# A linear-attention and two-MLP kernel: the first four jobs' odd key pairs turned by GpSimd, and their order on each engine changed

## The reference

```python
def _attn_ref(q, k, v, f_logit):            # (4, 8, 768, 48) each
    f = 1.0 / (1.0 + np.exp(-f_logit))
    for t in range(S):
        state = f[:, :, t, :, None] * state + np.einsum('bhd,bhe->bhde', k[:, :, t], v[:, :, t])
        y[:, :, t] = np.einsum('bhd,bhde->bhe', q[:, :, t], state)

def _moe_ref(x, w_in, w_out):               # (3072, 384) @ (384, 2048), and back
    r = np.maximum(x @ w_in, 0.0)
    return (r * r) @ w_out

def _moe2_ref(x, w_in, w_out):
    h = x @ w_in
    return (h * np.tanh(log1p(exp(h)))) @ w_out
```

## Time and profile before

| | |
|---|---|
| median of 3 runs | 886.29 us (885.81 to 890.02) |
| the profiled execution | 886.69 us, of which 885.0 us are the span from first to last instruction |
| PE busy | 874.3 us (99%) |
| DVE, ACT, POOL busy | 597.2, 594.8, 62.0 us |
| the chain that ended last | PE 98% |
| first instruction of `up1(0)` | 28.62 us from the span's start |
| granted TensorE clock | 1.000 |

### The profile page before, as it was taken

The page is one execution under the profiler, slowest core; times in us unless marked ns, Lnnn a source line. Parts: engine busy times, 40 slices in busy tenths (PEclk is TensorE's granted clock), DMA queues, the critical chain, the costliest instruction groups (busy, mean ns, idle before and its releaser), DMA issues.

```text
span 885.0 us, 16260 instructions
## 1 busy us (share of the span) xinstructions
PE 874.3 (99%) x6282; PEld 725.3 (82%) x6282; DVE 597.2 (67%) x1054; ACT 594.8 (67%) x1026; POOL 62.0 (7%) x71
## 2 busy tenths in 40 slices
PE   8899999999999999999999999999999999999998
PEld 7788888888888888888788888888888888888886
DVE  6879545445544444342244799999898898898886
ACT  6776655564546555544566787888887887877874
POOL 0222111111111111110000000000000000000000
PEclk9999999999999999999999999999999999999999
DMA  9644221122212111100233201001001001000100
GB/s 255 203 148 128 76 81 44 44 81 65 66 45 80 44 44 57 46 13 1 92 96 100 90 19 37 37 0 37 37 1 37 36 1 37 36 0 1 36 1 36
DMA packets 25090, 50.64 MB, mean 57 GB/s; under 512 B 2674, under 2 KB 3442, under 8 KB 25010
## 3 DMA queue, kind: packets, MB, share of 16 engines
q1 hardware_dynamic: 25010, 49.56, 18.0%
HBM read 40.11 MB, written 9.44 MB: 56 GB/s over the span
## 4 chain that ended last, share of the span: by engine, by line
PE 98%; DMA 1%; issue 0%; SPq 0%; ACT 0%; DVE 0%; ACTq 0%
PE ps L1069 45%; PE ps L1086 44%; PE ps L1043 2%; PE ps L1013 2%; PE ps L1039 2%; PE ps L991 1%; PE ps L1059 1%; DMA work<-fkq 1%; SPq L284 0%; PE ps L988 0%; PE ps L997 0%; SPq L297 0%; ACT work L497 0%; ACT work L538 0%; SPq L306 0%
## 5 line engine op out<-in xcount | busy, mean ns | idle before, releaser
L1069 PE MATMUL ps<-xs,w_hi 128*128 128x512 f32 x1152 | 359.3, 393 | 1.0 <-issue 1.0
L1069 PEld LDWEIGHTS ps<-xs,w_hi 128*128 128x128 f32 x1152 | 213.0, 188 | 45.0 <-issue 1.6
L1086 PE MATMUL ps<-g_hi,w_lo 128*128 128x512 f32 x576 | 224.1, 389 | 0.0
L1069 PE MATMUL ps<-xs,w_lo 128*128 128x512 f32 x576 | 224.1, 389 | 0.0
L1086 PE MATMUL ps<-g_hi,w_hi 128*128 128x512 f32 x576 | 224.1, 389 | 0.0
L1086 PE MATMUL ps<-g_lo,w_hi 128*128 128x512 f32 x576 | 224.1, 389 | 0.0
L829 DVE TENSOR_TENSOR g_lo<-gb,g_hi 128x512 fp32r<-128x512 f32 x96 | 68.1, 709 | 215.6 <-ACT gb L564 215.6
L559 ACT ACTIVATE rb<-ps 128x512 f32<-128x512 f32 x96 | 57.3, 597 | 161.0 <-PE ps L1069 161.0
L1069 PEld LDWEIGHTS ps<-xs,w_lo 128*128 128x128 f32 x576 | 108.1, 188 | 22.6
L1086 PEld LDWEIGHTS ps<-g_hi,w_hi 128*128 128x128 f32 x576 | 108.1, 188 | 22.5
L1086 PEld LDWEIGHTS ps<-g_hi,w_lo 128*128 128x128 f32 x576 | 108.1, 188 | 22.4
(11 more groups left out here) (82 smaller groups left out, 750.6 us busy)
## 6 DMA issues: line engine op xcount, KB each, us to landing
work<-fkq SPq DMA_DIRECT2D x68, 224.0 KB, 3.7
stage<-w SPq DMA_DIRECT2D x24, 384.0 KB, 3.1
work<-v_tok SPq DMA_DIRECT2D x22, 256.0 KB, 3.9
x_scratch<-yo SPq DMA_DIRECT2D x6, 768.0 KB, 3.8
xs<-x_scratch SPq DMA_DIRECT2D x6, 768.0 KB, 4.4
out<-work SPq DMA_DIRECT2D x17, 256.0 KB, 2.1
yo<-w SPq DMA_DIRECT2D x8, 384.0 KB, 4.6
work<-f_tok SPq DMA_DIRECT2D x4, 224.0 KB, 3.5
```

What stands on the lines that cost most here:

```text
L1069: ins = nc.tensor.matmul(bank, w[:, f, k * P:(k + 1) * P], xs[:, half, part, k, :], start=k == 0 and i == 0, stop=k == KT - 1 and i == 2)
L1086: ins = nc.tensor.matmul(ps[:, 5 + d, :], w[:, f, cols], g[:, slot, :], start=f == 0 and i == 0, stop=f == NF - 1 and i == 2)
```

## The change

What it does, by engine:

- PE: `keys(j)` of the first four jobs is four whole transposes; those of pairs 1 and 3 read `turned`, a copy of the pair with its halves swapped, and wait for `kt_turned`. `increments(j)` has two matmuls for each pair, of 64 and 48 columns, where it had four of 32 and 16 (for all 20 jobs that have increments). `idle_products` makes 2 and 1 matmuls of 384 moving columns, where it made 6 and 3 of 128. `scores(0)` goes ahead of `sums(2)`, `scores(1)` ahead of `sums(3)`, `scores(2)` ahead of `keys(2)` and `values(1)`, `increments(1)` ahead of `values(2)`.
- POOL: `turn(j)`, two copies of 112x2x64 elements for each of the four jobs, in `rb`. The second job's and later ones wait for `kT_done` of the job before, since `turned` is one buffer.
- ACT: `first_logarithm(2)` goes behind `first_decay(1)`; `keys_out(2)` and `keys_out(3)` go ahead of `weights_hi(0)` and `ends_out(2)`, and write in `eb`, so that they no longer wait for `kv_done`; `inverse_decay(4)` and `(5)`, which write over `eb`, wait for it instead.
- DVE: `first_cap(2)` goes behind `first_queries(0)`.

```diff
--- before.py
+++ after.py
@@ -34,7 +34,7 @@
     WF = 2 * DM
     NT = NF * NCH
     AHEAD = 4
-    IDLE = [6, 3]
+    IDLE = [(3, 3), (3,)]
     LIMIT = 8.0e16
     BOUND = 1.0e18
     CAP = 1.0e17
@@ -188,7 +188,7 @@
         names = """set_up zeroed st_zeroed const_ready causal_ready
             ft_exped ft_capped ft_logged sums_done m_ready
-            exped inv_f scanned logged p_ready ends_kept kt_ready gp_ready qp_ready qt_ready pc_ready
+            exped inv_f scanned logged p_ready ends_kept kt_ready kt_turned gp_ready qp_ready qt_ready pc_ready
             kT_done kT_out a_done a_out y_done kv_done s_added s_ready
             mx_kept mx_out mx_in mx_reduced flag_ready
             fsel_zeroed f_set_up f_loaded f_ready fv_loaded fkv_ready fst_ready fw_ready fy_done fy_out
@@ -239,11 +239,17 @@
         tri = rb[:, 0:C]
+        turned = rb[:, C:C + 2 * C].rearrange("p (n h t) -> p n h t", n=2, h=2)
         def f_rows(j):
             return (fb if j < 2 else eb)[:, j % 2, :, :].rearrange("p n t -> p (n t)")[:, 0:NP * R]
         def key_rows(j):
+            if j in (2, 3):
+                return eb[:, j % 2, :, :].rearrange("p n t -> p (n t)")[:, 0:NP * R].rearrange("p (n r) -> p n r", r=R)
             return ktT[:, j % 2, :, :]
         def v_rows(j):
@@ -480,6 +486,16 @@
                 nc.gpsimd.tensor_tensor(eb[0:R, j % 2, :, :], mb[0:R, j % 2, :, :], pb[0:R, j % 2, :, :],
                                         ALU.mult).then_inc(s_["gp_ready"], 1)
+            def turn(j):
+                pool.wait_ge(s_["kt_ready"], j + 1)
+                wait(pool, s_["kT_done"], j)
+                k = kt[0:R, j % 2, 1::2, :].rearrange("p n (h t) -> p n h t", h=2)
+                for h in range(2):
+                    nc.gpsimd.tensor_copy(turned[0:R, :, h, :], k[:, :, 1 - h, :]).then_inc(s_["kt_turned"], 1)
+            for j in range(B):
+                turn(j)
             for j in range(B, NJ):
                 decayed_keys(j)
                 residual(j)
@@ -514,6 +530,8 @@
                 act.wait_ge(s_["pc_ready"], j - 1)
                 act.wait_ge(s_["sums_done"], B)
                 act.wait_ge(f_in[j % 2], 16 * (j // 2 - 1))
+                if j < B + 2:
+                    act.wait_ge(s_["kv_done"], j - 1)
                 e = eb[0:R, j % 2, :, :]
                 nc.scalar.activation(e, fb[0:R, j % 2, :, :], ACT.Exp, scale=-1.0).then_inc(s_["exped"], 1)
                 act.wait_ge(s_["exped"], j - B + 1)
@@ -533,8 +551,6 @@
                 act.wait_ge(s_["kT_done"], j + 1)
                 if j >= B:
                     act.wait_ge(s_["kv_done"], min(j - 1, NJ - B))
-                elif j >= 2:
-                    act.wait_ge(s_["kv_done"], j - 1)
                 nc.scalar.activation(key_rows(j), ps_k(j), ACT.Copy).then_inc(s_["kT_out"], 1)
             def x1_hi(j):
@@ -650,9 +666,9 @@
             first_exponential(2)
             first_growth(0)
             first_decay(0)
-            first_logarithm(2)
             first_growth(1)
             first_decay(1)
+            first_logarithm(2)
             ends_out(0)
             first_exponential(3)
             first_growth(2)
@@ -664,15 +680,15 @@
             first_decay(3)
             keys_out(1)
             x1_hi(0)
+            keys_out(2)
             weights_hi(0)
             x1_hi(1)
+            keys_out(3)
             ends_out(2)
             ends_out(3)
             x1_hi(2)
             x1_hi(3)
             weights_hi(1)
-            keys_out(2)
-            keys_out(3)
             weights_hi(2)
             inverse_decay(4)
             for k in range(SPLIT):
@@ -901,9 +917,9 @@
             first_cap(0)
             first_cap(1)
-            first_cap(2)
             first_keys(0)
             first_queries(0)
+            first_cap(2)
             first_keys(1)
             first_queries(1)
             first_cap(3)
@@ -981,14 +997,13 @@
                     pe.wait_ge(s_["r1_ready"], 2)
                 if j == B + 1:
                     pe.wait_ge(s_["kT_out"], B + 1)
                 for n in (0, 2, 1, 3):
+                    k = kt[0:R, j % 2, n, :]
                     if j < B and n % 2 == 1:
-                        for at in (0, HC):
-                            ins = nc.tensor.matmul(ps_k(j)[at:at + HC, n, :], kt[0:R, j % 2, n, HC - at:C - at], ident[0:R, 0:R],
-                                                   start=True, stop=True, skip_group_check=True, tile_position=(0, at))
-                    else:
-                        ins = nc.tensor.transpose(ps_k(j)[:, n, :], kt[0:R, j % 2, n, :], ident[0:R, 0:R])
+                        if n == 1:
+                            pe.wait_ge(s_["kt_turned"], 2 * j + 2)
+                        k = turned[0:R, n // 2, :, :].rearrange("p h t -> p (h t)")
+                    ins = nc.tensor.transpose(ps_k(j)[:, n, :], k, ident[0:R, 0:R])
                 ins.then_inc(s_["kT_done"], 1)
             def sums(j):
@@ -1053,10 +1068,9 @@
                 else:
                     pe.wait_ge(s_["r1_ready"], begin[j + 1] + 1)
                 for n in range(NP):
-                    for i in range(4):
-                        lo, hi = Q * i, min(Q * i + Q, R)
-                        v0, v1 = VALUES[i // 2]
-                        ins = nc.tensor.matmul(ps_kv(j)[lo:hi, n, :], key_rows(j)[:, n, lo:hi], v_rows(j)[:, 2 * n + i // 2, v0:v1],
+                    for par, (lo, hi) in enumerate(ROWS):
+                        v0, v1 = VALUES[par]
+                        ins = nc.tensor.matmul(ps_kv(j)[lo:hi, n, :], key_rows(j)[:, n, lo:hi], v_rows(j)[:, 2 * n + par, v0:v1],
                                                start=True, stop=True, skip_group_check=True, tile_position=(0, lo))
                 ins.then_inc(s_["kv_done"], 1)
@@ -1144,31 +1158,32 @@
-            def idle_products(count, bank):
-                for i in range(count):
-                    nc.tensor.matmul(ps[:, bank, 0:P], ident[:, :], ident[:, :], start=True, stop=True, skip_group_check=True)
+            def idle_products(widths, bank):
+                for n in widths:
+                    nc.tensor.matmul(ps[:, bank, 0:n * P].rearrange("p (n t) -> p n t", t=P), ident[:, :],
+                                     ident[:, :].unsqueeze(1).to_broadcast([P, n, P]), start=True, stop=True, skip_group_check=True)
             pe.wait_ge(s_["const_ready"], 4)
             idle_products(IDLE[0], 6)
             sums(0)
             sums(1)
             idle_products(IDLE[1], 6)
+            scores(0)
             sums(2)
-            scores(0)
             keys(0)
+            scores(1)
             sums(3)
-            scores(1)
             keys(1)
             values(0)
+            scores(2)
             keys(2)
-            scores(2)
             values(1)
+            scores(3)
             keys(3)
-            scores(3)
             increments(0)
+            increments(1)
             values(2)
             values(3)
-            increments(1)
             increments(2)
             increments(3)
             for k in range(SPLIT):
```

## The result

The changed kernel is slower: 892.49 us median of 6 runs (891.16 to 893.47), beside 886.66 us of the kernel before (6 runs) on the same chip; ratio 1.0058 [1.0040, 1.0075]. The profiled execution took 892.25 us, of them 890.5 us of span. The forecast was 882.0, with 881.0 to 886.0. In all six runs the mean granted clock is 0.996 to 0.998.

What follows compares the result with a forecast made beforehand. TensorE's chain was taken as the bound, held ahead of `up1(0)` by instruction fetches and VectorE. `up1(0)` from 28.62 to 24.2 gives 4.4 us, so 881.9; with 0.1 for VectorE's slack 882.0, range 881.0 to 886.0.

Steps and rivals of the forecast that it cites:

- increments 64 to 32 by four: Instruction count ahead of `up1(0)`: broad increments in the first four jobs save 128 of the 966 instructions.
- I take 0.65: Two broad increments behind the last stall: 0.65 us, between 0.53 and 1.07, where 64 narrow matmuls took 1.07.
- a stall put down to issue, in `increments(2)`: Sign expected on TensorE ahead of `up1(0)`: a 1.5 us stall, 256 instructions behind one in `scores(3)`.
- 5.45 us from border to use: Second instruction fetch on TensorE: the block for `increments(2)` arrives 5.45 us after the one for `scores(3)`, at 23.55.
- the first rival: Instruction block comes later, each us delaying `up1(0)` by one; 9.7 us starts it at 28.5; 883.3 to 886; chance 0.22.
- the forecast's own sign of being wrong: Instruction queue ahead of `up1(0)`: the forecast is wrong if a packet starts over 4 us behind its border.
- The order: Scores moved ahead in the first jobs: `mask(3)` ends 2.5 us early, and this bound lets `up1(0)` go at 23.75.
- no fetch bound: Rival: third block in time, `up1(0)` waits for `x1_lo(3)` alone, at 23.75; gain 4.9 us, 881.4; chance 0.13.
- Keys whole: First four jobs' keys by whole transposes: 1.4 us of TensorE saved, but before VectorE waits, so none counted.
- POOL's copies: Turning keys in the first jobs: 0.5 us a copy, 1.0 a job, bounds 0.2 and 1.9; hidden at 1.0.
- ScalarE's wait for the keys: TensorE's 1.43 us wait for `keys_out(2)` and `(3)` ahead of `up1(0)`: gone, as the copies are through by 20.
- VectorE's shorter slack: First tile: `g1_lo(0)` ends at 30.5 to 30.7, `down1(0)` wants it at 30.5; 0.1 us counted.

Runs made afterwards that it cites:

- e1_loop_narrow: The changed kernel with four narrow increment matmuls for jobs 4 to 19, broad ones only for jobs 0 to 3: 886.39 us, 0.9998.
- e7_turned_alone: The kernel before with only the turned keys added (POOL's copies and four whole transposes): 886.29 us, 0.9998.
- e10_loads_alone: The kernel before with only the keys and queries of job 4 and weights of tile 3 held until increments(0) is done: 887.87 us, 1.0009.
- e8_three_loads_late: e1_loop_narrow with the loads of job 4's keys and queries and tile 3's weights held until increments(1) is done: 882.83 us, 0.9961.
- e3_loads_late: e1_loop_narrow with five loads (f, k, q of job 4 and two weight tiles) held until increments(1) is done: 884.70 us, 0.9973.
- e13_broad_loads_late: The changed kernel, broad increments in all jobs, with job 4's keys and queries and tile 3's weights held until increments(1) is done: 887.20 us, 1.0013.
- e5_more_idle: e1_loop_narrow with its three idle products of 384 columns cut into 25 of 64, 88 instructions more: 888.93 us, 1.0026.
- e12_narrow_all: The changed kernel with narrow increments in every job, the first four too: 888.40 us, 1.0009.
- e4_idle_narrow: e1_loop_narrow with nine idle products of 128 columns in place of three of 384, 24 instructions more: 886.98 us, 1.0006.
- e6_order_alone: The kernel before with the change's new order on all engines only; half-matmul keys, narrow increments and idle products as before: 887.49 us, 1.0009.

## Why the prediction was wrong

**The step that failed: "increments 64 to 32 by four".** The front part names the broad increments for all 20 jobs, and the sum has only the first four. Nothing was counted for the sixteen of the loop, and no rival had them. They cost 4.2 us, which is nearly all of the 4.3 us forecast as a gain. The row that gives it was in reach: 0.34 us for 32 narrow records in the chain of before. The half as many broad ones could have been bounded between 0.17 and 0.68 us, 2.7 us faster to 5.4 slower over sixteen jobs.

**The same term in the first jobs was mis-sized.** For two jobs "I take 0.65", out of 0.53 to 1.07. `increments(0)` and `(1)` took 1.06 us, at the upper bound: half the matmuls with twice the columns gave nothing. Behind the border 30 of the 32 records took 1.02 us at full clock in e1_loop_narrow: 0.4 us on the path.

**The fetch: the mechanism was right, the size was not.** 256 instructions to a block, the stalls at 449 and 705, and "a stall put down to issue, in `increments(2)`" came as told. 5.45 us from border to use became 7.05, which is the first rival, and the forecast's own sign of being wrong came with it: the packet started 4.5 us behind its border. I had given the rival 0.22, on the ground of one row; seven runs now give 5.5 to 9.1 us. It was 1.6 us too little here, and the first border ended 1.6 us later than counted (19.70, not 18.1): `scores(1)` started at 12.31 and not at 11.65, and 7.4 us and not 6.4 went by from there. With 1.0 us more in the increments (0.4 by their size, the rest by the clock) that is the way from 24.2 to 28.41. That the rival had `up1(0)` at 28.5 is luck: it took a fetch of 9.7 us for it. The Trainium skill (Runtime: NRT & Kernel Launch, Instruction fetch mechanics) says that a block is asked for while the one before it is executed, and that crossing its border is mostly hidden. The first half agrees with the traces (the second block is used 4.1 us and more after the first border); "mostly hidden" does not hold here, where seven profiled executions stand 1.1 to 4.4 us at one border. For PE's store this section of the Trainium skill has 128 KiB, which would be eight blocks, and also two lines of 16 KiB; the stalls fit two, and no run here shows the number directly.

**The clock was not in the sum.** A stall of 2.65 us or more was followed by the lower level in each of the four profiles that had one; 1.55 us before and 1.17 in e1_loop_narrow were not. The length alone does not tell: in e7_turned_alone the level fell behind a wait of 1.74 us, in e10_loads_alone (0.59 from 28 to 32 us) behind waits of 1.42 and 0.71 us, and before it stayed at 1.00 behind 1.55 and 1.43 us. In the changed kernel it cost 0.79 us at `up1(0)` and about 0.7 in the increments (1.74 us for the 30 records for which e1_loop_narrow took 1.02). So a late block costs more than its lateness.

**What held.** The order: without a stall `up1(0)` waits for `x1_lo(3)` and starts at 23.60, beside 23.75 in the rival "no fetch bound". Keys whole and POOL's copies: nothing, as e7_turned_alone has it. A copy took 0.4 to 0.6 us in the changed kernel and 0.27 at best in others (0.53 us for two in e7_turned_alone), about the 0.5 counted or less. ScalarE's wait for the keys is gone. VectorE's shorter slack is where the forecast put it, but larger: TensorE loses 0.9 us at `down1(0)`, which waits for `g1_lo(0)`, in e8_three_loads_late and e3_loads_late, and 0.1 was counted. (VectorE's "10.0 us of work" in that sum are 33.93 - 23.39 - 0.8 = 9.7; its end at 30.5 to 30.7 goes with the 9.7.) 1.2 us of `mask(3)` were lost to the first stall, which lasted to 19.70 and was counted to 18.1.

**What stays open.** The 0.55 us more of stall at the branch: e13_broad_loads_late has 1.05 there as before, so that it is not the order or the increments. Over the fourteen profiles the stall is 1.05 to 1.60 us, 1.5 or more in e5_more_idle, e10_loads_alone and e12_narrow_all too, with no edit that they share; what sets it is not known. The same section of the Trainium skill says that a taken branch breaks the sequential fetch, which agrees with the place; nothing here tests it. Why e1_loop_narrow has two heaps of runs 3.5 us apart is argued, not shown: only one of the lower heap was profiled. The stalls of 3.3 to 4.4 us with the fallen clock, in e4_idle_narrow, e6_order_alone and e12_narrow_all, are what the upper heap would look like, and the lower mean clock of six of its seven runs fits that. What makes the packet start later in one execution than in the next was not taken apart. Why 16 records of 64 and 48 columns take 0.60 us where 32 of 32 and 16 take 0.34 in the loop, but no more than those in the first jobs, was not taken apart.

## What to carry to other kernels

Count an edit in every place where its code runs, not only where the change is about; a quarter of a microsecond in a loop of sixteen ate all of the gain ahead of it (e13_broad_loads_late, 887.20 us). Where "issue" stalls stand 256 instructions of an engine's list apart, look at what the data queues move between the two borders: reordering only brings the engine to the border sooner, and the loads that aren't needed yet have to make room first. A new order and the freed queue were each worth nothing here, and 3.5 us together (882.83 us); try pairs before an edit is dropped.

## What the runs showed that was not expected

A block of 16 KB of instructions took at most 4.1 to 4.9 us from border to use where loads were held back (queue 48% busy in e8_three_loads_late), and 5.5 to 9.1 us where they were not and the engine stalled (95% in e1_loop_narrow). The difference is the wait for its one packet to start, though it is 1.4% of the traffic.

Fewer and broader small matmuls can be slower: 0.60 against 0.34 us for a job's increments in the loop. And cutting columns into narrower idle products made them dearer: 768 columns at the start took 5.38 us as twelve products (e5_more_idle) and 2.93 as two (changed kernel).
